# The inverse root of two tiles' norms, worked on four token columns and spread through DRAM

## What is computed

```python
attn_out = _attn_ref(r, k, v, w, u)          # a linear attention with a decaying state, 3072 tokens in all
x = attn_out.transpose(0, 2, 1, 3).reshape(B * S, H * D)
x = _moe_ref(x)                              # silu(x @ w_gate) * (x @ w_val) @ w_out, 384 -> 1536 -> 384
# second layer:
rms = np.sqrt(np.mean(x * x, axis=-1, keepdims=True) + 1e-06)
xn = x / rms * rms_g
g = xn @ w_gate
silu = g * (1.0 / (1.0 + np.exp(-g)))
val = xn @ w_val
return (silu * val @ w_out)
```

## Time and profile before

| | us |
|---|---|
| median of 3 runs | 995.81 |
| lowest and highest | 994.24, 995.89 |
| the profiled execution | 995.4 |
| its span in the trace | 993.5 |
| PE busy in it | 964.3 |
| DVE busy in it | 679.7 |

### The profile page before, as it was taken

The page is one execution under the profiler, slowest core; times in us unless marked ns, Lnnn a source line. Parts: engine busy times, 40 slices in busy tenths (PEclk is TensorE's granted clock), DMA queues, the critical chain, the costliest instruction groups (busy, mean ns, idle before and its releaser), DMA issues.

```text
span 993.5 us, 23903 instructions
## 1 busy us (share of the span) xinstructions
PE 964.3 (97%) x9426; PEld 797.2 (80%) x9426; DVE 679.7 (68%) x1074; ACT 404.3 (41%) x851; POOL 549.4 (55%) x441
## 2 busy tenths in 40 slices
PE   7989999999999999999999999999999999999998
PEld 5989988888888888888877777787888777878876
DVE  4786756576857756674419967788677799567760
ACT  4544343334333433433432454434633446344423
POOL 7598876566666565565233315678526787211134
PEclk7899999999999999999999999999999999999999
DMA  7554443535434343533142155443064441344201
GB/s 296 163 172 127 147 135 116 180 105 182 174 125 149 131 149 112 175 144 124 56 154 85 43 187 216 159 154 111 33 223 157 140 160 53 105 171 159 80 1 64
DMA packets 50495, 134.58 MB, mean 135 GB/s; under 512 B 6800, under 2 KB 10320, under 8 KB 50384
## 3 DMA queue, kind: packets, MB, share of 16 engines
q1 hardware_dynamic: 50384, 133.05, 38.7%
HBM read 106.78 MB, written 25.17 MB: 133 GB/s over the span
## 4 chain that ended last, share of the span: by engine, by line
PE 75%; POOL 7%; DVE 7%; issue 7%; DMA 1%; ACT 1%; POOLq 0%; SPq 0%; DVEq 0%; ACTq 0%
PE ps_down L883 7%; PE ps_down L885 6%; PE ps_down L884 6%; PE ps_val L883 6%; PE ps_val L885 6%; PE ps_val L884 6%; PE ps_gate L883 5%; PE ps_gate L885 5%; PE ps_gate L884 5%; PE ps_level L979 4%; PE ps_level L1184 2%; PE ps_level L1186 2%; PE ps_level L1185 2%; PE ps_val L1184 1%; PE ps_val L1044 1%
## 5 line engine op out<-in xcount | busy, mean ns | idle before, releaser
L1964 POOL TENSOR_TENSOR h_lo<-h_raw,h_hi 128x512 fp32r<-128x512 f32 (+1 forms) x84 | 113.2, 1348 | 220.4 <-ACT h_hi L1291 211.6
L883 PE MATMUL ps_down<-h_hi,down_hi 128*128 128x512 f32 (+1 forms) x360 | 134.9, 375 | 1.7 <-DVE room_c L1818 0.9
L885 PE MATMUL ps_down<-h_lo,down_hi 128*128 128x512 f32 (+1 forms) x360 | 132.6, 368 | 0.0
L884 PE MATMUL ps_down<-h_hi,down_lo 128*128 128x512 f32 (+1 forms) x360 | 132.6, 368 | 0.0
L1567 DVE TENSOR_TENSOR h_raw<-h_raw,ps_val 128x512 f32<-128x512 f32 (+1 forms) x84 | 51.0, 608 | 88.0 <-PE ps_val L885 79.9
L1291 ACT ACTIVATE h_hi<-h_raw 128x512 fp32r<-128x512 f32 (+1 forms) x84 | 47.9, 571 | 150.1 <-DVE h_raw L1567 150.0
L883 PE MATMUL ps_gate<-x_hi,up_weights 128*128 128x512 f32 (+1 forms) x252 | 94.7, 376 | 1.6 <-ACT h_raw L1285 1.6
L883 PE MATMUL ps_val<-x_hi,up_weights 128*128 128x512 f32 (+1 forms) x249 | 91.1, 366 | 4.2 <-DVE h_raw L1567 2.5
L885 PE MATMUL ps_gate<-x_lo,up_weights 128*128 128x512 f32 (+1 forms) x252 | 91.7, 364 | 0.0
L884 PE MATMUL ps_gate<-x_hi,up_weights 128*128 128x512 f32 (+1 forms) x252 | 91.5, 363 | 0.0
L885 PE MATMUL ps_val<-x_lo,up_weights 128*128 128x512 f32 (+1 forms) x249 | 90.0, 362 | 0.0
(11 more groups left out here) (293 smaller groups left out, 2402.7 us busy)
## 6 DMA issues: line engine op xcount, KB each, us to landing
ring<-sums_dram SPq DMA_DIRECT2D x72, 640.0 KB, 4.8
r_block<-in_r_blk_dram SPq DMA_DIRECT2D x22, 768.0 KB, 5.1
chunk_in<-in_a_t_dram SPq DMA_DIRECT2D x24, 512.0 KB, 3.7
chunk_in<-in_a_n_dram SPq DMA_DIRECT2D x22, 384.0 KB, 4.3
sums_dram<-sum_lo SPq DMA_DIRECT2D x24, 320.0 KB, 3.1
staging<-in_weights_dram SPq DMA_DIRECT2D x18, 384.0 KB, 3.9
raw<-in_blocks_dram SPq DMA_DIRECT2D x8, 576.0 KB, 5.5
sums_dram<-sum_hi SPq DMA_DIRECT2D x12, 320.0 KB, 2.6
```

The lines of the kernel that those rows point to most:

```text
L883: nc.tensor.matmul(dst, w_hi, x_h, start=first, stop=False)
L884: nc.tensor.matmul(dst, w_lo, x_h, start=False, stop=False)
L885: return nc.tensor.matmul(dst, w_hi, x_l, start=False, stop=last)
L1964: nc.gpsimd.tensor_tensor(h_lo[:, f % 3, 0:WIDTH[t]], h_raw[:, f % 2, 0:WIDTH[t]], h_hi[:, f % 3, 0:WIDTH[t]].bitcast(F32), ALU.subtract). ...
```

## The change

The inverse roots of second-layer tiles 0 and 1 are worked out on 128x4 instead of 128x512. After the ones matmul, ScalarE copies one partition of the sums (1x512) to SBUF (`copy_row`). A DMA turns that row of 512 into 128 partitions of 4 (`turn_sums`). VectorE does the 15 instructions of guess and three Newton steps on 128x4 (`invert`), a DMA stores the 512 results in a new DRAM tensor, and a second one, issued when the first has landed, reads them back to all 128 partitions (`spread_inverse`). `norm_x` is as before, with its wait on that last DMA.

The slots move too. `NORM_AT` goes from (6, 7) to (8, 9), and with it the squares, their sums and the ones matmuls. `invert` stands in slot 12 for both tiles, `norm_x` in 16 and 17 (14 and 20 before). `SUM_AT` begins at 18 and spreads the 11 sums to slot 26; `MADE_AT` begins at 19, one part per slot to 33 (22 to 34 before). The store of the inverses and its reads stand in SP's queue behind the first ring.

```diff
-NORM_AT = (6, 7)
-SUM_AT = [21 + i * 6 // len(SUMMED) for i in range(len(SUMMED))]
-MADE_AT = [22 + i * 13 // NPROD for i in range(NPROD)]
+NORM_AT = (8, 9)
+INVERSE_AT = (12, 12)
+NORM_X_AT = (16, 17)
+SUM_AT = [18 + i * 9 // len(SUMMED) for i in range(len(SUMMED))]
+MADE_AT = [19 + i * 16 // NPROD for i in range(NPROD)]
...
+            def turn_sums(k):
+                sp.wait_ge(row_copied, k + 1)
+                sp.dma_start(turned(k)[:, 0, :], norm_of(k)[1][0:1, :].rearrange("o (p j) -> o p j", j=TOK // P))\
+                  .then_inc(turned_in[k], 16)
+
+            def spread_inverse(k):
+                sp.wait_ge(inverse_done, k + 1)
+                sp.dma_start(inverse_dram[k].rearrange("(p j) -> p j", j=TOK // P), turned(k)[:, 1, :]).then_inc(inverse_stored, 16)
+                sp.wait_ge(inverse_stored, 16 * (k + 1))
+                sp.dma_start(norm_of(k)[0], inverse_dram[k].unsqueeze(0).broadcast_to([P, TOK])).then_inc(inverse_in[k], 16)
...
                 load_ring(g)
+                if g == 0:
+                    for k in range(2):
+                        turn_sums(k)
+                    for k in range(2):
+                        spread_inverse(k)
                 if g < PAIRS - 2:
                     load_down2(g + 2)
...
+            def copy_row(k):
+                act.wait_ge(norm_summed, k + 1)
+                nc.scalar.activation(norm_of(k)[1][0:1, :], bank[6 + k][0:1, :], ACT.Copy).then_inc(row_copied, 1)
...
+                            if s == NORM_AT[k] + 1:
+                                copy_row(k)
...
+            def invert(k):
+                half, y, z = turned(k)[:, 0, :], turned(k)[:, 1, :], turned(k)[:, 2, :]
+                done = [14 * k]
+                def chain(ins):
+                    done[0] += 1
+                    ins.then_inc(root_step, 1)
+                    dve.wait_ge(root_step, done[0])
+                dve.wait_ge(turned_in[k], 16)
+                chain(nc.vector.tensor_scalar(half, half, 0.5 / DM, 0.5e-6, ALU.mult, ALU.add))
+                chain(nc.vector.tensor_scalar(y.bitcast(I32), half.bitcast(I32), 1, None, ALU.logical_shift_right))
+                chain(nc.vector.tensor_scalar(y.bitcast(I32), y.bitcast(I32), -1.0, float(0x5F3759DF - 0x400000), ALU.mult, ALU.add))
+                for i in range(3):
+                    chain(nc.vector.tensor_tensor(z, y, y, ALU.mult))
+                    chain(nc.vector.tensor_tensor(z, z, half, ALU.mult))
+                    chain(nc.vector.tensor_scalar(z, z, -1.0, 1.5, ALU.mult, ALU.add))
+                    last = nc.vector.tensor_tensor(y, y, z, ALU.mult)
+                    if i < 2:
+                        chain(last)
+                last.then_inc(inverse_done, 1)
...
                 if k < 2:
-                    dve.wait_ge(newton_dve, 12 * (k + 1))
+                    dve.wait_ge(inverse_in[k], 16)
...
                         for k in range(2):
-                            if s == NORM_AT[k] + 1:
-                                norm(k)
-                            for i in range(3):
-                                for part in range(2):
-                                    if s == NORM_AT[0] + 2 + 6 * k + 2 * i + part:
-                                        newton_step(k, i, part)
-                            if s == NORM_AT[0] + 8 + 6 * k:
+                            if s == INVERSE_AT[k]:
+                                invert(k)
+                            if s == NORM_X_AT[k]:
                                 norm_x(k)
```

More of the change, by code:

```diff
@@ L377, in build @@
 def build(nc, a_t, a_n, r_blk, w_t, u_t, w_blk, w_last, weights, down2, blocks2, rms_g, level_mask, fine_mask, block_mask,
-          identity, v_first, out, x2_dram, sums_dram):
+          identity, v_first, out, x2_dram, sums_dram, inverse_dram):
     with ExitStack() as ctx:
@@ L500, in build, with turned @@
         norm_room = over("norm_room", [P, 2, TOK], F32, "chunk_in", 2 * FREED * TOK)
-        norm_room1 = over("norm_room1", [P, 3, TOK], F32, "chunk_in", (FREED - 3) * TOK)
+        norm_room1 = over("norm_room1", [P, 2, TOK], F32, "chunk_in", (FREED - 2) * TOK)
         def norm_of(k):
             if k == 1:
-                return norm_room1[:, 0, :], norm_room1[:, 1, :], norm_room1[:, 2, :]
+                return norm_room1[:, 0, :], norm_room1[:, 1, :], None
             return norm_room[:, 0, :], norm_room[:, 1, :], half_mean[:, :]
+        def turned(k):
+            return half_mean[:, k * 12:k * 12 + 12].rearrange("p (x j) -> p x j", x=3)
         ones = over("ones", [P, P], F32, "pow_nat")
@@ L670, in build @@
         newton = sem("newton")
-        newton_dve = sem("newton_dve")
+        row_copied = sem("row_copied")
+        turned_in = [sem("turned_in0"), sem("turned_in1")]
+        root_step = sem("root_step")
+        inverse_done = sem("inverse_done")
+        inverse_stored = sem("inverse_stored")
+        inverse_in = [sem("inverse_in0"), sem("inverse_in1")]
         k_weighed = sem("k_weighed")
@@ L1145, in step @@
                         if chain_of(p) == 0:
-                            pe.wait_ge(norm_step, 1 * 3 + 1)
+                            pe.wait_ge(row_copied, 2)
                         elif value == 0:
@@ L1158, in step @@
                             if r + 1 < ROUNDS and q - 2 < 2:
[L1160 removed]
+                                pe.wait_ge(norm_step, (2 * r + q - 2) * 3 + 1)
                         elif r == 0:
@@ L1737, in chain @@
                     ins.then_inc(norm_step, 1)
-                    dve.wait_ge(norm_step, 3 * k + n)
-                place = bank[6 + k] if k < 2 else bank[BANKS[k // 2 - 1][1 + k % 2][4]]
+                    dve.wait_ge(norm_step, 3 * (k - 2) + n)
                 a, b, half = norm_of(k)
                 dve.wait_ge(norm_summed, k + 1)
-                chain(nc.vector.tensor_scalar(half, place, 0.5 / DM, 0.5e-6, ALU.mult, ALU.add), 1)
+                chain(nc.vector.tensor_scalar(half, bank[BANKS[k // 2 - 1][1 + k % 2][4]], 0.5 / DM, 0.5e-6, ALU.mult, ALU.add), 1)
                 chain(nc.vector.tensor_scalar(a.bitcast(I32), half.bitcast(I32), 1, None, ALU.logical_shift_right), 2)
                 chain(nc.vector.tensor_scalar(a.bitcast(I32), a.bitcast(I32), -1.0, float(0x5F3759DF - 0x400000), ALU.mult, ALU.add), 3)
-            def newton_step(k, i, part):
-                a, b, half = norm_of(k)
-                n = 12 * k + 4 * i + 2 * part
-                if part == 0:
-                    dve.wait_ge(ones_done, 2)
-                    reach(dve, newton_dve, n)
-                    nc.vector.tensor_tensor(b, a, a, ALU.mult).then_inc(newton_dve, 1)
-                    dve.wait_ge(newton_dve, n + 1)
-                    nc.vector.tensor_tensor(b, b, half, ALU.mult).then_inc(newton_dve, 1)
-                else:
-                    dve.wait_ge(newton_dve, n)
-                    nc.vector.tensor_tensor(b, one_half[:, :].broadcast_to([P, TOK]), b, ALU.subtract).then_inc(newton_dve, 1)
-                    dve.wait_ge(newton_dve, n + 1)
-                    nc.vector.tensor_tensor(a, a, b, ALU.mult).then_inc(newton_dve, 1)
             def norm_x(k):
@@ L2037, in newton_step @@
                 if part == 0:
-                    pool.wait_ge(norm_step, 3 * k + 3)
+                    pool.wait_ge(norm_step, 3 * (k - 2) + 3)
                     reach(pool, newton, n)
@@ L2251 @@
     sums = nc.dram_tensor("sums_dram", (GROUPS, 2, P, GROUP), F32, kind="Internal").ap()
-    build(nc, *args, out, x2, sums)
+    inverse = nc.dram_tensor("inverse_dram", (2, TOK), F32, kind="Internal").ap()
+    build(nc, *args, out, x2, sums, inverse)
     got = run_bass_kernel_spmd(nc, [arrays], core_ids=[0]).results[0]["out_dram"]
```

1 line of the change is left out of this document (removed).

## The result

| | before | after |
|---|---|---|
| median, us (8 runs each, taken together) | 995.24 | 989.01 |
| lowest and highest | 993.28, 996.87 | 986.59, 991.80 |
| the profiled execution | 995.4 | 987.0 |
| its span | 993.5 | 985.1 |
| slot 0 of the last tile to the second layer, in the trace | 87.29 | 81.98 |

The ratio is 0.9938, with a 95% interval of 0.9920 to 0.9956: faster, by 0.4 to 0.8%. The last row is measured from the first silu of the last tile to the first silu of the second layer.

A forecast was written before the change was run, and what follows sets the result against it. TensorE was taken to bound the kernel, so only its idle time in the first layer's last tile counts: 1.89 + 3.40 = 5.29 us off 995.81, nothing added, gives 990.5 us. The 8-in-10 range was 989.3 to 993.3.

The forecast's parts named there:

- four stalls: TensorE's waits in the first layer's last tile: one on silu, 1.89 us, three on VectorE's product, 3.40 us together.
- Part 1: Squares two slots later in the last first-layer tile, so TensorE's wait on silu at gate 2 goes: gain 1.89 us.
- Part 2: Small Newton chain gives VectorE 15 to 18 us back, so products are on time: gain up to 3.40 us.
- Part 3: The new chain and its DMA waits, from slot 10 on: all hidden, nothing added to the tile.
- One hold by GpSimd: In the small chain on VectorE, GpSimd's subtraction may hold one instruction once, for up to 1.7 us.
- The read back: DMA of the inverses from DRAM to all partitions, 256 KB: 2.3 us, after a store of about 2.0.
- `norm_x` waiting past 537 for its DMA: Sign of being wrong: VectorE waits that long for the inverse, showing as a TensorE wait in slots 17 to 29.
- The hand: Time in hand before TensorE wants the banks that VectorE's products empty: about 2 us in each place.
- Carried undiminished to the end: From the second layer's start to the end: the tile's whole gain of 5.29 us is kept.
- Lateness comes back: Rival, chance 0.25: VectorE's products late again in the tile, 1.9 to 2.2 us of the gain lost, 992.5 us.
- The long round trip: Rival, chance 0.06: store and read of inverses take 8.0 us each, 12 us of stall, kernel slower at 1002.5.
- Nothing much won: Rival, chance 0.07: first stall and some late products in the tile stay, under 2 us won, 994.5 us.

The follow-up runs named there:

- c4: Changed kernel with squares, their adds and ones matmuls back in slots 6 and 7: median 991.97 us, ratio 0.9967 to the kernel before, tile 83.90.
- d3: Changed kernel with the old slot tables for norm_x of tile 1, sums and parts: 987.52 us in one profiled execution, tile 81.98.
- d4: Kernel before with two tiny ScalarE copies (1x3) added in slots 9 and 10: 996.16 us in one profiled execution, tile 87.27.
- c1: Kernel before, run again unchanged as a control: median 995.38 us of 12 runs, ratio 0.9997 to its other runs, tile 87.32.
- d2: Changed kernel with six Newton steps instead of three: 992.67 us in one profiled execution, tile 86.64.
- d5: Changed kernel with six DMA reads added behind the last output, each waited for: 2 KB row to all partitions 3.1 us, rows apart 2.6.
- d1: Changed kernel with each inverse read back twice, one read after the other: 996.62 us in one profiled execution, tile 87.36.
- c3: Kernel before with squares, adds and ones matmuls two slots later, inverse roots still on 128x512: median 995.31 us, ratio 0.9995, tile 86.74.

## Why the prediction was right, and where it was not

**What bounds the kernel, and the sum: right.** 5.29 us were forecast for the tile, and 87.29 - 81.98 = 5.31 measured. PE's idle time was read off in four stalls, each with its releaser named, and all four are gone. The second layer's first matmul came at 570.97, with the 3.44 that is 574.41; 574.4 was forecast.

**Part 1: right.** The squares start at 505.42 + 3.44 = 508.86 (508.9 forecast) without a wait, and c4 gives 1.92 for the stall (1.89).

**Part 2: right.** VectorE is busy 41.13 of 53.2 us (38 to 42), it got 59.38 - 43.88 = 15.5 us back (15 to 18), a step takes 0.20, and c4 gives 3.39 (3.40). Taking the value near the low bound, for the reason that nothing stands in the gap, was the right choice.

**Part 3: right in the outcome, with terms mis-sized.** One hold by GpSimd did come, and cost 1.0 (up to 1.7 allowed). The instruction caught was L1786, a multiplication and addition with constants and a single SBUF input. The prediction had counted, by the rule of the Trainium skill ("SBUF — State Buffer", section "SBUF: two separate sides"), only the 18 multiplications of two tensors as open to it. That was half of the rule: the same section of the Trainium skill names instructions in a two-port mode as well, and its page "VectorE: DVE Perf Modes", section "Mode 2×_2P — use both read ports for one tensor", gives that mode to instructions of one tensor input from SBUF, float32 too. Whether L1786 ran in it no row shows; that such an instruction is held, the trace shows (1.15 us). Beside the 18, eight of the 30 are float32 with one input.
The read back was forecast at 2.3 us and took 4.0 and 5.4; the stores took 1.4 and 2.6 (2.0). The inverse of tile 0 was in at 535.7, where 533.9 to 535.6 were forecast, that of tile 1 at 541.2 instead of 538 to 539.5. The step that gave these terms took both prices from rows of other shapes, from 1.6 to 2.6 us: the "small ones" that it sets beside the 320 KB store are a load and a copy within SBUF, and no row has a small store or a read of one DRAM row to all partitions. It also left out what else is under way, the first read for the second store and the down weights for the second read. One of the prediction's own signs of being wrong came up: "`norm_x` waiting past 537 for its DMA". That of tile 1 waited until 541.2, but the wait of TensorE that was to follow did not come. The hand took it up: it was put at 2 us, and 1.9, 1.7 and 1.4 remained at the three products.
The third piece of down weights went out at 532.71 + 3.44 = 536.15 (536), and no silu waited for it. The old tables give the same tile (d3).

**Carried undiminished to the end: wrong by 0.35.** Second layer to the end is 405.15 instead of 404.80 in the profiled pair. Of 5.31 us 4.96 are left. d4, with its tile as long as before, ties the loss to the two added ScalarE instructions; what they do to the last high part stays open.

**The predicted time and its range.** 990.5 was forecast, and 989.01 came out, 0.3 us below the low end of 989.3. The failed step is the low end, "the forecast with the runs' own scatter below it (1.6 us between lowest and highest, so about 1.2)". Three runs cannot show that scatter: the eight of after alone are 5.2 us apart, those of before 3.6.

The 1.49 us between 990.5 and 989.01 have two parts. The starting value, a median of three runs (995.81), was 0.57 above that of eight (995.24). And the medians differ by 6.23 instead of 5.29, which no part of the mechanism gives: the traces show 4.96. The other two sets give 4.7 and 3.1. By the means, weighted with the numbers of runs, the three sets give 4.7 together (95% interval 3.8 to 5.5, by resampling the runs within each set), which holds the 4.96 and not the 6.23. So the first set shows more than the change is worth, as far as is known by chance: the 25 runs of the changed kernel lie between 985.8 and 993.6 with a deviation of 2.1 and a median of 990.5, and of medians of eight drawn from them one in ten is as low as 989.01. The 68 runs of the kernel before, c1 with them, lie between 991.4 and 999.2, deviation 1.7. That the middle of the forecast is also the median of these 25 is in part luck: the start made it 0.57 too high, the missing loss at the end 0.35 too low, and the sets differ in their level. Nineteen in twenty such medians of eight lie between 988.3 and 991.7, so a low end of about 988 would have been right.

Where the scatter sits was looked for in the traces. The profiled execution of after came to the tile 3.44 us sooner than that of before, with the same work up to there. Two of the stretches in which they part, for the kernel before (first PE's busy time, third number from the right the clock):

```profile
72.00:82.00 10.00, 9.25 (x181) 8.89 (x178) 6.82 (x11) 2.09 (x6) 9.81 (x9) 0.83 0.35 112
...
144.00:154.00 10.00, 8.26 (x148) 6.72 (x141) 4.60 (x11) 2.86 (x9) 2.37 (x3) 0.83 0.30 100
```

and after:

```profile
72.00:82.00 10.00, 9.57 (x231) 9.33 (x232) 8.41 (x13) 3.41 (x10) 10.00 (x9) 1.00 0.47 148
...
144.00:154.00 10.00, 9.14 (x113) 7.58 (x106) 5.71 (x13) 4.50 (x11) 4.09 (x4) 1.00 0.49 159
```

In the second stretch the kernel before has a wait on nothing that the profile shows:

```profile
PE ps_val L1055 <- issue: 0.9, 1, 0.9
```

This wait is absent in after and d3, 0.6 in d2 and d5, and between 0.9 and 2.0 in the other nine traces. In the first four the clock stays at 1.00 over this stretch, and they reach the tile between 498.0 and 499.6; in the nine it is 0.66 to 0.83, and they reach it between 501.4 and 504.4. So most of this scatter goes with an issue wait that comes and goes, and with the clock that falls behind it. Why it comes is open. All four with a wait of 0.6 or none are kernels with the small chain, but five others with it are among the nine; whether the change has a part in it is not shown, and by the interval of the timed runs (3.8 to 5.5 for the whole) little room is left for it.

**The rivals.** *Lateness comes back* did not happen, though the read was as slow as it supposed for the two together (5.4 and 8.0 us against its 7). It asked for the small step at 0.30 as well, and it took the two round trips one after the other. They overlapped in part: from the first store's issue to the second `norm_x` are 537.73 - 526.84 = 10.9 us instead of 14, and the product that it had 2 us late was 1.4 early. *The long round trip* was priced at stall time alone. It would have been nearer than it looked: by d1, an inverse of tile 1 that comes 5.9 us later (`norm_x` at 547.95, less the 4.29 by which that tile starts later, against 537.73) already eats the gain. In both the price of a stall was too low: each of the three stalls of 2.8 us and more that the runs made cost a further 1.4 to 1.8 in slow matmuls behind it. *Nothing much won* had no row for it and did not come; it is what c3 gives, with part 1 alone.

## What to carry to other kernels

Where a second engine is late as well, removing the first stall alone may only move the waiting to that engine's next place, and gather short stalls into a long one that costs more than their sum, as in c3; take the load off that engine together with the stall. A serial chain of tiny instructions is priced by its interval from start to start (0.20 us here), plus one hold for each instruction of GpSimd that starts beside it (1.0 us here), and whoever stands behind it in the queue decides whether that is free. A round trip through DRAM is priced with what is under way beside it (3.1 us for the read alone, 4.0 and 5.4 in the kernel). And the length of the stretch that the change touches repeated to 0.05 us in every trace of the same order, where single executions differed by more than 6: judge an edit of half a per cent by the stretch, and make the range for a median from the scatter of many runs.

## What was not expected of the hardware

- TensorE's clock behind a stall. After idle times of 2.68, 2.72 and 3.51 us (c3, d2, d1) six to eight matmuls ran at the lower level, 0.43 from start to start; after those of 1.29 and 1.59 in the kernel before the clock stayed at 1.00. What decides between is not shown.
- VectorE's instruction of one SBUF input on 128x4 took 1.15 us, to the end of GpSimd's subtraction, though it reads only 2 KB.
- A 2 KB row read to all 128 partitions took 3.1 us alone, and 4.0 to 5.4 in the kernel; 256 KB from rows apart 2.6.
- A 2 KB store issued while such a read was under way landed with the read: 2.6 us in the changed kernel and 3.1 in d1 (536.93 to 540.01, `norm_x` on the read at 539.93), instead of 1.4.
- With two more ScalarE instructions in the first layer's last tile, the last high part of the program, some 460 us later, starts 0.28 us later.
